# Slots re-laid to 128 rows through DRAM, batches written out, and POOL's scatters between the accumulating DMAs of part 0 and of part 1

## The reference

```python
def _attn_ref(q, k, v):                       # (8, 8, 576, 64)
    k_p = k.reshape(B, H, Sp, 8, D).mean(axis=3)
    v_p = v.reshape(B, H, Sp, 8, D).mean(axis=3)
    scores = scale * np.matmul(q, k_p.transpose(0, 1, 3, 2))
    ...
    return np.matmul(attn, v_p)
def _moe_ref(x, w_gate, w_noise, noise, w1, w2):   # x (4608, 512), 8 experts, F = 1024
    noisy_logits = x @ w_gate + np.log1p(np.exp(x @ w_noise)) * noise
    top2 = np.argpartition(-noisy_logits, 2, axis=1)[:, :2]
    ...
            h = np.maximum(x[mask] @ w1[e], 0.0)
            out[mask] += top2_w[mask, k, None] * (h @ w2[e])
def _moe2_ref(x, w_in, w_out):                # 512 -> 2048 -> 512
    h = x @ w_in
    return (h - np.tanh(h)) @ w_out
```

## Time and profile before

| | |
|---|---|
| median of 3 runs | 1995.78 us (1995.45 to 1996.97) |
| profiled execution | 2000.64 us, its span 1999.1 us |
| mean granted clock of TensorE | 0.982 of full speed |
| busy: PE, PE's weight loads, DVE, ACT, POOL | 1904.6, 1732.7, 999.7, 820.0, 532.8 us |
| DMA | 107722 packets, 152.42 MB, mean 76 GB/s |

### The profile page before, as it was taken

One profiled execution on the slowest core, in us unless ns is written; L12 is line 12 of the kernel. 1 busy time (PEld: TensorE's weight loads), 2 busy tenths in 40 slices (PEclk: granted clock), 3 DMA queues, 4 the chain that ended last, 5 costly groups with the idle time before them and its releaser, 6 DMA issues.

```text
span 1999.1 us, 36280 instructions
## 1 busy us (share of the span) xinstructions
PE 1904.6 (95%) x13072; PEld 1732.7 (87%) x13073; DVE 999.7 (50%) x1928; ACT 820.0 (41%) x1720; POOL 532.8 (27%) x532
## 2 busy tenths in 40 slices
PE   5988778999999999999999969999999999999999
PEld 5887777898999999999998958999899999999998
DVE  3878652231313132131313137777766677777765
ACT  4877632332323132232324135444444444444444
POOL 2255443221221112211122122222222232223222
PEclk9999878999999999999999979999999999999999
DMA  8778612341313122131314130000000110000000
GB/s 206 169 163 166 148 30 94 125 141 42 136 52 126 42 83 95 50 129 42 126 49 140 42 126 32 32 31 31 31 31 31 52 43 31 31 31 31 31 31 22
DMA packets 107722, 152.42 MB, mean 76 GB/s; under 512 B 50624, under 2 KB 75328, under 8 KB 104864
## 3 DMA queue, kind: packets, MB, share of 16 engines
q1 hardware_dynamic: 81600, 98.98, 16.0%
q0 software_dynamic: 26080, 52.90, 9.9%
HBM read 111.52 MB, written 40.33 MB: 76 GB/s over the span
## 4 chain that ended last, share of the span: by engine, by line
PE 82%; DMA 6%; issue 5%; DVE 3%; POOL 2%; ACT 2%; POOLq 0%; another core or an unknown queue 0%; DVEq 0%; ACTq 0%; SPq 0%
PE banks L775 13%; PE banks L774 13%; PE banks L773 13%; PE banks L764 13%; PE banks L766 13%; PE banks L765 13%; DMA slot_row<-row_id,slot_i 5%; PE banks L754 3%; POOL slot_row L503 1%; DMA k_raw<-in_k 1%; PE banks L641 0%; ACT pr L920 0%; DVE w_lo L1306 0%; PE banks L800 0%; PE banks L802 0%
## 5 line engine op out<-in xcount | busy, mean ns | idle before, releaser
L764 PE MATMUL banks<-x_hi,w_hi 128*128 128x256 f32 x2304 | 640.1, 278 | 7.2 <-DVE x_lo L1325 6.3
L766 PE MATMUL banks<-x_hi,w_lo 128*128 128x256 f32 x2304 | 639.4, 278 | 0.0
L765 PE MATMUL banks<-x_lo,w_hi 128*128 128x256 f32 x2304 | 639.4, 278 | 0.0
L773 PE MATMUL banks<-w_hi,h_hi 128*128 128x512 f32 x1184 | 468.2, 395 | 9.0 <-issue 5.5
L775 PE MATMUL banks<-w_hi,h_lo 128*128 128x512 f32 x1184 | 466.7, 394 | 0.0
L774 PE MATMUL banks<-w_lo,h_hi 128*128 128x512 f32 x1184 | 463.7, 392 | 0.0
L764 PEld LDWEIGHTS banks<-x_hi,w_hi 128*128 128x128 f32 x2304 | 436.0, 189 | 10.3 <-DVE x_lo L1325 7.3
L765 PEld LDWEIGHTS banks<-x_lo,w_hi 128*128 128x128 f32 x2304 | 435.9, 189 | 2.4
L766 PEld LDWEIGHTS banks<-x_hi,w_lo 128*128 128x128 f32 x2304 | 435.8, 189 | 0.0
L604 POOL TENSOR_SCALAR large<-u_sq 128x512 uint8<-128x512 f32 x144 | 222.4, 1545 | 585.3 <-ACT u_sq L1079 317.8
L1332 DVE SCALAR_TENSOR_TENSOR h_lo<-banks,h_hi 128x512 fp32r<-128x512 f32 x144 | 99.3, 691 | 373.2 <-ACT h_hi L1008 197.8
(11 more groups left out here) (156 smaller groups left out, 2093.9 us busy)
## 6 DMA issues: line engine op xcount, KB each, us to landing
w_raw<-in_moe_w SPq DMA_DIRECT2D x32, 1024.0 KB
y<-y_rows SPq DMA_DIRECT2D x18, 1024.0 KB, 5.0
q_sb<-in_q SPq DMA_DIRECT2D x32, 288.0 KB
x_rows<-x_sb SPq DMA_DIRECT2D x64, 144.0 KB
out_x<-y_sb SPq DMA_DIRECT2D x36, 256.0 KB, 2.1
k_raw<-in_k SPq DMA_DIRECT2D x16, 288.0 KB
v_raw<-in_v SPq DMA_DIRECT2D x16, 288.0 KB
k_raw<-in_k POOLq DMA_DIRECT2D x16, 288.0 KB
```

Of the source, the lines that this page charges most:

```text
L764: pe.matmul(part, hi, x_hi[:, c, :], start=(c == 0), stop=False)
L765: pe.matmul(part, hi, x_lo[:, c, :], start=False, stop=False)
L766: mm = pe.matmul(part, lo, x_hi[:, c, :], start=False, stop=(c == NC - 1))
L773: pe.matmul(p_y[m][:, :], hi, w_hi[par][:, o:o + DM], start=(j == 0), stop=False)
```

## The change

The slots of a batch are stored to DRAM by SP (store_slots, slot_flat) and read back as 128 partitions of WAY = 9 (load_slots, slot_w, two buffers); the row numbers are relaid the same way once, at the start (row_flat, row_w). POOL scatters nine times 128 rows. The loops of batches 2 to 6 are written out on all engines. All nine scatters of batch b-2 stand between POOL's adds of part 0 and of part 1 of batch b+1. part5 waits for the store of the last slots instead of for scatters. The first y_sent is raised at the start, SP's load of rows_all comes ahead of the first weights of expert 1, and DVE makes the early tokens at head 4 of batch 7.

```diff
+    WAY = 2 * S // 128
+    slot_flat = nc.dram_tensor("slot_flat", (B, 2 * S), i32).ap()
+    row_flat = nc.dram_tensor("row_flat", (B, 2 * S), i32).ap()
...
+        def landed(b, i):
+
+            return 16 * (((b + 1) * WAY + 1 - i) // 2)
...
+            def store_slots(b):
+                sp.wait_ge(routed, b + 1)
+                sp.dma_start(slot_flat[b:b + 1, :].rearrange("o (p k) -> p (o k)", k=2 * TT),
+                             slot_i[:, :, :].rearrange("p i t -> p (i t)")).then_inc(slot_out, 16)
+
+            def load_slots(b):
+                sp.wait_ge(slot_out, 16 * (b + 1))
+                if b >= 2:
+                    for i in range(2):
+                        sp.wait_ge(scattered[i], landed(b - 2, i))
+                sp.dma_start(slot_w[b % 2][:, :], slot_flat[b:b + 1, :].rearrange("o (p n) -> p (o n)", n=WAY)).then_inc(slot_in[b % 2], 16)
...
@@ SP, body @@
                 if not (isinstance(b, int) and b < 2):
+                    store_slots(b - 2)
                     store_route(b - 2)
                 if not is_first(b):
                     store_x(b - 1, 3)
+                if not (isinstance(b, int) and b < 2):
+                    load_slots(b - 2)
...
-            with sp.Fori(2, B - 2) as b:
+            for b in range(2, B - 2):
                 body(b, ahead=True)
...
+            store_slots(B - 2)
             store_x(B - 1, 2)
+            load_slots(B - 2)
             store_x(B - 1, 3)
             store_route(B - 2)
+            store_slots(B - 1)
+            load_slots(B - 1)
             store_route(B - 1)

+            sp.wait_ge(counted, 1)
+            for i in range(2):
+                sp.wait_ge(scattered[i], landed(B - 1, i))
+            sp.dma_start(rows_all[:, 0:COLS], slot_row.rearrange("(p n) o -> p (n o)", n=COLS)).then_inc(rows_in, 16)
             for c in range(2):
                 sp.wait_ge(split_lo, 4 * (c + 3))
                 load_w(c, w_src(1, c))
...
@@ POOL @@
+            pool.sem_inc(y_sent, 1)
...
-            def scatter(b, choices=(0, 1)):
-
-                if 0 in choices:
-                    pool.wait_ge(routed, b + 1)
-                settle(pool)
-                for i in choices:
-                    for t in range(TT):
-                        n = i * TT + t
-                        if n >= 2:
-                            pool.wait_ge(scattered[n % 2], b * 16 * TT + 16 * (n // 2))
-                            settle(pool)
-                        pool.indirect_dma_start(slot_row, bass.IndirectOffsetOnAxis(ap=slot_i[:, i, t:t + 1], axis=0),
-                                                row_id[:, i * TT + t:i * TT + t + 1], None).then_inc(scattered[n % 2], 16)
+            def scatter(b):
+
+                pool.wait_ge(slot_in[b % 2], 16 * (b // 2 + 1))
+                for n in range(WAY):
+                    k = b * WAY + n
+                    wait(pool, scattered[k % 2], 16 * (k // 2))
+                    pool.indirect_dma_start(slot_row, bass.IndirectOffsetOnAxis(ap=slot_w[b % 2][:, n:n + 1], axis=0),
+                                            row_w[:, b, n:n + 1], None).then_inc(scattered[k % 2], 16)

             add_values(0, 0)
+            pool.dma_start(row_flat.rearrange("b (p k) -> p b k", k=2 * TT), row_all[:, :, :]).then_inc(row_flat_out, 16)
             add_keys(0, 1)
             add_values(0, 1)
+            pool.wait_ge(row_flat_out, 16)
+            pool.dma_start(row_w[:, :, :], row_flat.rearrange("b (p n) -> p b n", n=WAY)).then_inc(row_w_in, 16)
...
                 if back:
-                    scatter(b - 2, (0,))
+                    scatter(b - 2)
                 if not is_last(b):
                     add_keys(b + 1, 1)
                     add_values(b + 1, 1)
-                if back:
-                    scatter(b - 2, (1,))
...
-            with pool.Fori(2, B - 1) as b:
+            for b in range(2, B - 1):
                 body(b)
...
             scatter(B - 1)
-            pool.sem_inc(y_sent, 1)
             send(0, rows_a, 0)
...
@@ DVE @@
-                for i in range(2):
-                    wait(dve, scattered[i], b * 16 * TT)
-                dve.tensor_copy(row_id[:, :], row_all[:, bass.ds(b, 1), :].rearrange("p o t -> p (o t)"))
+                wait(dve, slot_out, b * 16)
...
-                    if last and s == 1:
+                    if last and s == 4:
                         dve.wait_ge(rows_a_in, 16)
```

More of the change, by code:

```diff
@@ L131, in attention_moe_ffn @@
         row_all = sb("row_all", [TP, B, 2 * TT], i32, c=a_ctx)
-        row_id = sb("row_id", [TP, 2 * TT], i32, c=a_ctx)
+        row_w = sb("row_w", [128, B, WAY], i32, c=a_ctx)
+        slot_w = [sb(f"slot_w{i}", [128, WAY], i32, c=a_ctx) for i in range(2)]
         tri_f = sb("tri_f", [TP, TP], c=a_ctx)
@@ L198, in attention_moe_ffn @@
         consts, dve_consts, loads0 = sem("consts"), sem("dve_consts"), sem("loads0")
-        zeroed = sem("zeroed")
+        zeroed, row_flat_out, row_w_in = sem("zeroed"), sem("row_flat_out"), sem("row_w_in")
+        slot_out, slot_in = sem("slot_out"), [sem(f"slot_in{i}") for i in range(2)]
         q_in = [sem(f"q_in{i}") for i in range(PAIRS)]
@@ L241, in settle @@
             eng.sem_inc(settled, 1)
[L243 to L248, removed]
         POOL_CONSTS, DVE_CONSTS = 9, 9
@@ L355, in store_x @@
                                  x_sb[:, :, u, 0:D]).then_inc(x_out[p], 16)
+            def store_slots(b):
[8 more added lines that the diff above has]
+                sp.dma_start(slot_w[b % 2][:, :], slot_flat[b:b + 1, :].rearrange("o (p n) -> p (o n)", n=WAY)).then_inc(slot_in[b % 2], 16)
             def store_route(b):
-                sp.wait_ge(routed, b + 1)
                 for i in range(2):
@@ L402, in _ @@
                 load_w(c, w_src(1, c))
-            sp.wait_ge(counted, 1)
-            for i in range(2):
-                sp.wait_ge(scattered[i], 16 * TT * B)
-            sp.dma_start(rows_all[:, 0:COLS], slot_row.rearrange("(p n) o -> p (n o)", n=COLS)).then_inc(rows_in, 16)
             sp.wait_ge(route_out, 32 * B)
@@ L519, in body @@
                     add_values(b + 1, 1)
-                if back:
-                    scatter(b - 2, (1,))
             body(0, back=False)
             body(1, back=False)
-            with pool.Fori(2, B - 1) as b:
+            for b in range(2, B - 1):
                 body(b)
             for i in range(2):
-                pool.wait_ge(scattered[i], 16 * TT * (B - 3))
+                pool.wait_ge(scattered[i], landed(B - 4, i))
             pool.dma_start(rows_a[:, :], slot_row.rearrange("(p n) o -> p (n o)", n=COLS)[:, 0:AHEAD * SUB]).then_inc(rows_a_in, 16)
@@ L552, in _ @@
             scatter(B - 1)
-            pool.sem_inc(y_sent, 1)
             send(0, rows_a, 0)
             for i in range(2):
-                pool.wait_ge(scattered[i], 16 * TT * B)
+                pool.wait_ge(scattered[i], landed(B - 1, i))
             for p in range(PAIRS):
@@ L736, in _ @@
             body(1)
-            with pe.Fori(2, B - 1) as b:
+            for b in range(2, B - 1):
                 body(b)
@@ L989, in _ @@
             body(1)
-            with act.Fori(2, B - 1) as b:
+            for b in range(2, B - 1):
                 body(b)
@@ L1310, in _ @@
             body(1)
-            with dve.Fori(2, B - 1) as b:
+            for b in range(2, B - 1):
                 body(b)
```

1 line of the change is left out of this document (added).

## The result

The changed kernel takes 2004.82 us in the median of five runs (2003.21 to 2007.31), the kernel before 1996.18 beside it (1995.45 to 2001.16): ratio 1.0039, 95% interval 1.0024 to 1.0054, so 8.6 us slower. A ratio is the time over that of the kernel before on the same chip. Two more sets of executions, on two chips, gave 1.0040 [1.0026, 1.0053] and 1.0041 [1.0028, 1.0054]. The forecast was +16.5: the sign is right, the size double.

The account below looks back on a forecast made before the run. The prediction took a new circle through POOL's scatters and key add to bound the batches: +23.9 us, less 7.4 in the last stretch, net +16.5 on 1995.8, 2012.3 us. Its own range was 1999 to 2032, with rivals 1989 to 2036.

Parts of the forecast that it names:

- Leg (a): From slot_i to the first scatter, through SP's store and load of the slots: 7.0 us, ends 5.5 and 9.8.
- Leg (b): Nine scatters until POOL is free for the add of part 1: 15.6 us, ends 12.3 and 20.1.
- Leg (c): POOL's add of the part 1 keys until it has landed: 5.5 us, ends 4.9 and 6.4.
- Leg (d): DVE's work from the landed keys (k_raw) to slot_i of the next batch: 6.9 us.
- The last stretch: From slot_i of batch 5 to PE's turn to block 2: 84.0 us instead of 91.4, a gain of 7.4.
- The POOL path: Slot_i of batch 7, store and load, nine quiet scatters, then first send to the turn: 81.9 us from batch 5's slot_i.
- PE's path: From slot_i of batch 5: start of block 0 31.2, block 0 26.1, block 1 24.3; together 81.5 us.
- Written out at nothing: Writing out the loops on five engines costs 0, since the gap between unwaiting scatters is 0.30 us either way.
- the circle: Slots, store and load, nine scatters, key add, DVE, next slots: 35.0 us a batch; five periods 175.0 against 151.1, +23.9.
- the circle that does not bind: Rival: period 29.5 us, five periods 147.5 against 151.1, kernel faster at 1982.3 us; chance 0.17.
- the longer stretch: Rival: slower scatters and late keys give batches of about 40 us, five periods +48.9, total 2041.7; chance 0.13.
- the wash: Rival: batch period 31 to 32.5 us, its cost given back by the tail; chance 0.08.

Follow-up runs that it names:

- the tail edits alone: Kernel before with only y_sent raised at the start and the early tokens made at head 4 of batch 7: 2003.80 us, 1.0031.
- The same kernel: Changed kernel with the first y_sent back behind the last scatters: 2018.01 us, 1.0097, on one chip; 2005.73 us, 1.0029, on another.

## Why the forecast was right in sign and double in size

**Leg (a)**, 7.0: right. 97.63 - 91.15 = 6.5 in the first. The store took 4.16 and the load 1.77; the load is held by the store's landing there, and in the next batch by the x stores ahead of it in SP's list. On the rule of the Trainium skill cited there ("DMA: Bandwidth & Descriptors", anatomy of one DMA, about 2.0 us): the page gives it for DMAs that GpSimd issues, and the slots go by SP. The slot loads landed in 1.8 to 2.4 us, near it all the same, the stores in 2.1 to 4.2. The adds of keys, which POOL does issue, took 4.3 to 8.0, far from it.

**Leg (b)**, 15.6: 112.03 - 97.63 = 14.4 in the first, 13.4 to 16.4 in the five. **Leg (c)**, 5.5: 4.75 in the first, 4.3 to 4.7 in the next three, 8.05 in the last (248.05 to 256.10), where I had one value. **Leg (d)**, 6.9: 124.23 - 116.78 = 7.45. Sum of the first 33.1, of the fifth 35.4; five of them 172.4 where I had 175.0. This term, +23.9, came out at +21.4, and 175.4 and 172.9 in the two repeats. DVE's idle time, forecast about 9.3 per batch, is 8.0 to 9.9. That the place of the scatters makes it is shown by moving them: 172.4 to 138.6. So the mechanism of this term was right.

**The last stretch is the term that was mis-sized**: 84.0 forecast, 74.5 measured (76.8 and 75.4 in the repeats), a gain of 16.9 instead of 7.4. By its steps: block 0 starts 291.28 - 263.58 = 27.7 after slot_i of batch 5 (31.2 forecast), it takes 24.9 (26.1), block 1 21.9 (24.3). The POOL path, which I let decide, did not bind: slots 3.5 instead of 5.0 and nine scatters 322.77 - 311.31 = 11.5 instead of 12.3, a scatter every 1.27 us without waiting for a landing, and PE found the rows of block 2 there. The 2 us for weight loads in the way did not show at the turn. So of the 9.5 us, 7.1 are the three steps of PE's path (3.5, 1.2 and 2.4), 2.0 the weight loads, and 0.4 that I took POOL's 81.9 instead of PE's 81.5. What I carried over wrongly for PE and DVE were durations: the same two stretches, from slot_i of batch 5 to that of 6 and from there to that of 7, took 28.0 (4.13 of it a wait) and 26.1 us before, and 22.2 and 22.0 after (21.9 and 23.8, 21.5 and 23.6 in the repeats). The granted clock of PE was 0.74 and 0.75 in those stretches before, 0.91 and 0.92 after. These are windows of before:

```profile
242.00:270.00 28.00, 20.42 (x167) 19.30 (x165) 18.21 (x74) 15.67 (x50) 13.20 (x15) 0.74 0.30 68
270.00:296.00 26.00, 22.69 (x144) 21.49 (x145) 16.46 (x68) 5.89 (x12) 11.63 (x12) 0.75 0.13 24
```

A low clock carried over from the stall ahead is not the reason. After, PE stood idle for longer there (no matmul from 249 to 256, and a clock of 0.50 until 264), and the stretches behind it still ran at 0.91. With the scatters last, the 18 us ahead of slot_i of batch 5 ran at 1.00, and the two stretches still took 24.5 and 24.2. Before, the clock was back up between the two low times, as the same part cut in three shows:

```profile
244.00:264.00 20.00, 15.38 (x137) 14.44 (x135) 14.84 (x58) 12.40 (x43) 10.24 (x11) 0.84 0.34 74
264.00:284.00 20.00, 13.73 (x73) 13.17 (x74) 8.89 (x32) 3.74 (x7) 9.97 (x11) 0.52 0.17 33
284.00:296.00 12.00, 12.00 (x91) 11.17 (x90) 9.23 (x47) 3.45 (x7) 4.38 (x5) 1.00 0.01 0
```

The clock is at 0.52 from 264 to 284, and in the changed kernel at 0.98 from 264 to 280. Part5's wait for the scatters lies inside the low time (265.7 to 269.9), but doesn't explain it by itself: PE had already stood idle for 2.65 us ahead of 265.29, for ACT's pT, and in the kernel with POOL's loop alone written out that wait is 1.02 us, and the two stretches still take 25.7 and 24.3. So the step that failed is this: I took the 4.13 us wait out, and left the rest of both stretches and of block 0 at the one price that a single trace showed. With part5's wait taken out they took 23.9 and 26.1 there, 24.6 and 24.3 in the kernel with POOL's list written out, 24.5 and 24.2 with the scatters last, and 21.5 to 22.2 and 22.0 to 23.8 in the changed kernel. That a lower clock and a longer stretch mostly stand together is what the rows show; no run holds everything else and changes the clock, so how much of the 9.5 us is the clock's stays open.

**Written out at nothing** was wrong on the kernel before, by 10 us, with ACT and DVE's lists the cause. Its reason, the same 0.30 us gap between scatters, was sound for POOL (0.9999) and said nothing of the other engines. But it is no further term to add: the 2.6 us between the two profiles are already whole without it, and what writing out does to the changed kernel's circle, whose nine scatters also wait for landings (22.3 us), was not measured. The kernel before written out (1.0051) is no faster than the changed one (1.0039 to 1.0041), so of the 8.6 us the loops alone could be all. Its five periods are 163.3, so against the 151.1 of the loops 12 us are there without any of the other edits, where the circle costs 21.4. The changed kernel with its loops kept wasn't tried; that share is open.

**The accounting**: 16.5, less 2.5 for the circle, less 9.5 for the last stretch, less 1.9 for the start and what lies behind the turn, plus 6.1 by which the two profiled executions stand off their medians, is 8.7, the measured 8.6. The 6.1 are no effect of the change that a row shows: the traces alone would have made it +2.6, so that 8.6 lies no further from 16.5 is luck in part. The prediction had named the case itself: period right and total not, then the tail is off. The rivals: the circle that does not bind is refuted (DVE waits in every batch), the longer stretch too (34.5 a period, not 40), the wash came nearest of them in time, though its period did not: at 34.5, the tail gave back 16.9 of the 21.4 us that the circle cost.

## What to carry to other kernels

When a batch's DMAs are put into one engine's list, ask of each what stands behind it and who waits for that: the same nine scatters made the five periods 34 us longer ahead of the last add than behind it. A stall that goes may return as another wait (the tail edits alone gained nothing and measured 6 us slower). And a stretch with its wait taken out is not known to 0.1 us: the two above took 50.0 us in one trace of the kernel before, 48.9 in another with the same work, and 44.3 to 45.8 after, so give it a range and not one value. Don't cost the writing-out of a loop at nothing from one engine's gaps, and time a control beside every variant on the same chip.

## What the runs showed of the hardware that was not expected

- The loops of ACT and DVE written out make the kernel before slower, 1.0034 [1.0020, 1.0049]; those of POOL, SP and PE give 0.9999, 0.9999 and 1.0012 (PE's in two groups, 1995.2 to 1999.6 us and 2005.2 to 2008.4). With ACT's and DVE's, POOL waits 59.2 us for landings of scatters instead of 48.0.
- Scatters of 128 rows in a quiet stretch issue every 1.27 us, POOL 0.97 of it, and did not wait for the landing of the one two before; a pair in 2.54 us, against the 2.85 of a pair of 96 rows before.
- The store of 4.5 KB of slots landed in a median of 2.8 us with nine scatters ahead of the adds of part 1, and of 7.1 us with six.
- The same kernel was 1.0097 and 1.0029 of before on two chips, the slower one with idle times of PE of 0.3 to 1.1 us that the profile puts down to nothing, in a straight list of matmuls.
